# Retention attention and two MLPs on one core: POOL loads the decay matrix, chunks load in halves, w_in tiles move to the first pass

## What is computed

```python
for b in range(nb):                       # blocks of 64 tokens
    intra = (qb @ kb.T * Dmask) @ vb      # Dmask[i, j] = lam ** (i - j) for i >= j
    inter = (qb * lam_pow) @ kv_state
    out[:, :, sl] = intra + inter
    kv_state = lam_block * kv_state + (kb * rev_pow).T @ vb
x = out                                   # (1536, 512)
h = x @ w_in;  g = np.maximum(0.01 * h, h);  x = g @ w_out
out = ((x @ w1) * (x @ w2)) @ w3 @ moe2_w_out
```

## Time and profile before

| | |
|---|---|
| median of 3 runs | 555.33 us (554.99 to 555.40) |
| the profiled execution | 555.02 us, span 553.1 us |
| PE busy | 546.3 us (99%), 2930 matmuls |
| DVE, ACT, POOL busy | 192.1, 155.4, 31.4 us |
| granted clock of PE | 1.00 |
| attention | to about 91 us of the span |
| moved by DMA | 39.7 MB |

### The profile page before, as it was taken

How to read it: one execution, slowest core, us unless ns; L and a number is a source line. 1 busy time by engine, 2 the same in 40 slices (tenths; PEclk the granted TensorE clock), 3 DMA queues, 4 the chain that set the end, 5 groups by cost and what they waited for, 6 DMA issues and landing times.

```text
span 553.1 us, 7821 instructions
## 1 busy us (share of the span) xinstructions
PE 546.3 (99%) x2930; PEld 448.6 (81%) x2930; DVE 192.1 (35%) x295; ACT 155.4 (28%) x267; POOL 31.4 (6%) x42
## 2 busy tenths in 40 slices
PE   8999999999999999999999999999999999999997
PEld 6788887888888888888888888788888888888885
DVE  4585664544342422222534444311111111111111
ACT  5232423434232322222433433311112111130111
POOL 6332420000000000000000000000000000000000
PEclk9999999999999999999999999999999999999999
DMA  7997773323111000000113210000002000020002
GB/s 267 361 370 261 242 274 115 115 89 102 57 39 38 1 0 0 0 0 0 30 47 99 92 39 0 1 1 1 0 1 76 0 0 0 0 77 0 1 0 76
DMA packets 17257, 39.71 MB, mean 72 GB/s; under 512 B 1856, under 2 KB 2888, under 8 KB 15696
## 3 DMA queue, kind: packets, MB, share of 16 engines
q1 hardware_dynamic: 15728, 29.63, 16.1%
q10 hardware_dynamic: 1472, 9.72, 4.7%
q0 software_dynamic: 32, 0.01, 0.0%
HBM read 34.10 MB, written 5.25 MB: 71 GB/s over the span
## 4 chain that ended last, share of the span: by engine, by line
PE 94%; DMA 2%; POOL 1%; DVE 1%; ACT 1%; issue 0%; SPq 0%; ACTq 0%
PE hid L629 16%; PE hid L630 16%; PE hid L631 16%; PE acc L629 13%; PE acc L630 13%; PE acc L631 13%; PE acc L716 2%; PE hid L665 2%; DMA stage<-weights 1%; PE acc L710 1%; POOL pow_row L328 1%; PE hid L730 1%; DMA pow_dram<-pow_row 0%; POOL pow_two L330 0%; DMA pow_two<-lam 0%
## 5 line engine op out<-in xcount | busy, mean ns | idle before, releaser
L629 PE MATMUL hid<-xy_hi,wa_hi 128*128 (+1 forms) x384 | 149.5, 389 | 0.0
L631 PE MATMUL hid<-xy_hi,wa_lo 128*128 (+1 forms) x384 | 149.4, 389 | 0.0
L630 PE MATMUL hid<-xy_lo,wa_hi 128*128 (+1 forms) x384 | 149.4, 389 | 0.0
L410 ACT ACTIVATE g<-hid 128x512 f32<-128x512 f32 (+1 forms) x72 | 43.1, 598 | 261.3 <-PE hid L631 261.3
L629 PE MATMUL acc<-g_hi,wb 128*128 128x512 f32 x286 | 111.4, 390 | 0.3 <-DVE g_lo L503 0.3
L630 PE MATMUL acc<-g_lo,wb 128*128 128x512 f32 x286 | 111.3, 389 | 0.0
L631 PE MATMUL acc<-g_hi,wb 128*128 128x512 f32 x286 | 111.3, 389 | 0.0
L629 PEld LDWEIGHTS hid<-xy_hi,wa_hi 128*128 128x128 f32 x384 | 72.1, 188 | 15.1 <-issue 0.2
L630 PEld LDWEIGHTS hid<-xy_lo,wa_hi 128*128 128x128 f32 x384 | 72.1, 188 | 15.0
L631 PEld LDWEIGHTS hid<-xy_hi,wa_lo 128*128 128x128 f32 x384 | 72.1, 188 | 14.9
L568 DVE TENSOR_TENSOR g<-g,hid 128x512 f32<-128x512 f32 (+1 forms) x48 | 33.0, 687 | 122.2 <-ACT g L410 122.2
(11 more groups left out here) (75 smaller groups left out, 298.8 us busy)
## 6 DMA issues: line engine op xcount, KB each, us to landing
stage<-weights SPq DMA_DIRECT2D x72, 256.0 KB, 2.8
qkv<-attn ACTq DMA_DIRECT2D x9, 1024.0 KB, 6.2
qkv<-attn SPq DMA_DIRECT2D x3, 1024.0 KB, 7.3
outT<-stage SPq DMA_DIRECT2D x11, 256.0 KB, 2.1
stage<-w_dram SPq DMA_DIRECT2D x8, 256.0 KB, 2.6
w_dram<-g SPq DMA_DIRECT2D x4, 256.0 KB, 3.3
w_dram<-w_out SPq DMA_DIRECT2D x4, 256.0 KB, 3.5
decay<-pow_dram SPq DMA_DIRECT2D x1, 512.0 KB, 4.1
```

The lines of the kernel that those rows point to most:

```text
L410: nc.scalar.mul(g[:, n % 2, :], hid[:, n % 2, 0, :], factor).then_inc(scaled, 1)
L629: nc.tensor.matmul(out, w_hi, a_hi, start=first, stop=False)
L630: nc.tensor.matmul(out, w_hi, a_lo, start=False, stop=False)
L631: return nc.tensor.matmul(out, w_lo, a_hi, start=False, stop=final)
```

## The change

It has three parts. POOL waits for its own store of the powers and issues the load of `decay`; SP neither waits for it nor issues the load. A chunk comes in two loads, its transposed q and k (`q_and_k_loaded`) and its k and v (`values_loaded`), and those who read one part wait for that one; SP's written order takes the halves between the weights. And `W_IN_AT` puts 3 tiles of w_in into attention, behind chunks 9, 10 and 11, in place of 8, behind chunks 3 to 10; 13 are left to the first pass.

```diff
-W_IN_AT = [0, 0, 0, 1, 1, 1, 1, 1, 1, 1, 1, 0]
+W_IN_AT = [0, 0, 0, 0, 0, 0, 0, 0, 0, 1, 1, 1]
...
+        def chunk_parts(c):
+            u = c % ATTN_RING
+            return [(qkv[:, u, QT:KC, :], attn[c][:, QT:KC, :], q_and_k_loaded[u]),
+                    (qkv[:, u, KC:VC + 1, :], attn[c][:, KC:VC + 1, :], values_loaded[u])]
...
-            def load_chunk(c):
-                sp.dma_start(qkv[:, c, :, :], attn[c]).then_inc(chunk_loaded[c], 16)
-
-
-            for w in range(STAGE - 1):
+            def load_part(c, part):
+                to, source, loaded = chunk_parts(c)[part]
+                sp.dma_start(to, source).then_inc(loaded, 16)
+
+
+            before_scores = len(w34_tiles(0, FIRST_34))
+            for w in range(before_scores):
                 load_weight(w)
-            load_chunk(0)
-            for w in range(STAGE - 1, len(EARLY_34)):
+            load_part(0, 0)
+            for w in range(before_scores, len(EARLY_34)):
                 load_weight(w)
-            wait_then_step(pow_stored, 16)
-            every_shift = bass.AP(pow_dram, 0, [[1, P], [2 * CHUNK, H], [1, CHUNK]])
-            sp.dma_start(decay[:, :, :], every_shift).then_inc(decay_loaded, 16)
-            load_chunk(1)
+            load_part(0, 1)
+            load_part(1, 0)
             next_block = len(EARLY_34) + len(tiles_at(0))
             for w in range(len(EARLY_34), next_block):
                 load_weight(w)
-            load_chunk(2)
+            load_part(1, 1)
+            load_part(2, 0)
+            load_part(2, 1)
...
             pool.dma_start(pow_dram.ap(), pow_row[:, :]).then_inc(pow_stored, 16)
+            pool.wait_ge(pow_stored, 16)
+            every_shift = bass.AP(pow_dram, 0, [[1, P], [2 * CHUNK, H], [1, CHUNK]])
+            pool.dma_start(decay[:, :, :], every_shift).then_inc(decay_loaded, 16)
...
-                pool.wait_ge(chunk_loaded[u], 16 * (c // ATTN_RING + 1))
+                pool.wait_ge(values_loaded[u], 16 * (c // ATTN_RING + 1))
...
                 if c % CPB > 0:
+                    pool.wait_ge(q_and_k_loaded[u], 16 * (c // ATTN_RING + 1))
...
-                    act.dma_start(qkv[:, c % ATTN_RING, :, :], attn[c + ATTN_RING]).then_inc(chunk_loaded[c % ATTN_RING], 16)
+                    for to, source, loaded in chunk_parts(c + ATTN_RING):
+                        act.dma_start(to, source).then_inc(loaded, 16)
...
-                pe.wait_ge(chunk_loaded[u], 16 * (c // ATTN_RING + 1))
+                pe.wait_ge(q_and_k_loaded[u], 16 * (c // ATTN_RING + 1))
...
                 pe.wait_ge(masked, 2 * c + 2)
+                pe.wait_ge(values_loaded[u], 16 * (c // ATTN_RING + 1))
```

More of the change, by code:

```diff
@@ L180, in build @@
         q_pow_copied = sem("q_pow_copied")
-        chunk_loaded = [sem(f"chunk_loaded{i}") for i in range(ATTN_RING)]
+        q_and_k_loaded = [sem(f"q_and_k_loaded{i}") for i in range(ATTN_RING)]
+        values_loaded = [sem(f"values_loaded{i}") for i in range(ATTN_RING)]
         staged = [sem(f"staged{i}") for i in range(STAGE)]
```

## The result

The changed kernel takes 561.47 us (median of 4 runs, 561.31 to 562.05) against 555.27 us for the kernel before in the same comparison: a ratio of 1.0117, 95% interval 1.0101 to 1.0133. It is 1.2% slower. Its profiled execution took 561.33 us with a span of 559.2 us, 6.1 us more than before. "No change" was wrong, and the range ended at 560.0.

A forecast was written before the change was run, and what follows sets the result against it. PE's busy time bounds the kernel (546.3 of 553.1 us), with one 1.04 us stall in reach. The terms, -1.04 + 0.88 = -0.16 us, carried to the median of 555.33, gave 555.2 us, range 554.1 to 560.0.

The forecast's parts named there:

- No change: Whole kernel: the verdict that a measurement would not tell it from the kernel before, about 0.2% (1.1 us); chance 0.48.
- Part 1: SP no longer waits for the powers, so PE's whole stall before product 16 goes: -1.04 us.
- Part 2: POOL issues the decay load; it lands at 18.85 and stalls PE before chunk 0's value products: +0.88 us.
- The store: POOL's store of the powers to DRAM, ahead of the decay load: taken to land at 13.45 as before.
- The start: Fixed part of POOL's decay load besides its transfer: 2.7 us, as POOL's nearly empty store took.
- the share: Decay load beside SP's queue: an even share of bytes, 0.52 MB at half of 396 GB/s, 2.65 us.
- The clock: PE's granted clock: a stall of several us could lower it; not priced, left in the upper end.
- my formula: PE's stall before chunk 0's value products equals the decay landing less 17.97, one for one; with it -1.04 us.
- Rival 2: Decay load crawls piece by piece behind SP's rows, stalling PE: up to +6.1 us, 561.4 us; chance 0.27.
- Rival 3: POOL writes the decay load's 1024 pieces slowly: 4.3 us, +0.8, 556.1 us; at 8 us 559.8; chance 0.15.
- Part 3: Chunks loaded in halves, with more loads on SP and ACT and pieces of 4 instead of 8 KB: 0.
- Part 4: Five w_in tiles leave attention for the first pass, PE waiting for neither: 0.

The follow-up runs named there:

- a2: The kernel before with only the w_in tiles moved (3 in attention, 13 in the first pass): 554.93 against 554.95 us, ratio 0.9999.
- d1: The kernel before with weight 10 loaded ahead of chunk 1, behind the decay load on SP: 554.33 against 554.86 us, ratio 0.9994 (0.9985 to 1.0003).
- f1: The kernel before with POOL issuing the decay load and SP held until it has landed: 559.91 us in a single execution.
- b4: The changed kernel with ACT, behind its first ten hi parts, issuing the decay load in place of POOL: 564.9 us (1.0156 to 1.019).
- a4: The kernel before with only the chunks in halves, decay load still on SP: 559.03 us (1.0054 to 1.0095).
- c3: a4 with each half stored in one piece in DRAM: 554.77 against 554.86 us, ratio 1.0001 (0.999 to 1.0012).
- b1: The changed kernel with SP held for the powers' store before it loads q and k of chunk 1: 558.52 us.
- b2: The changed kernel with SP held for the powers' store only before k and v of chunk 1: 563.39 us.

## Why the prediction was wrong

**Part 1 was right in direction.** No wait for `w_ring` is left at 22 us, the engines are full from 12 to 15 us (408 GB/s), and weight 10 lands by 16.6 (I had counted about 13, but no product wanted it before 22). But its 1.04 us was the size in one trace. How early PE is differs from trace to trace: its matmuls on the powers start anywhere between 10.95 and 11.85 us in 14 traces of different kernels. Before, product 16 waited for a tile that came by its own clock, so a later start only shortened that wait: a2 starts 0.67 us later than before and waits 0.2 instead of 1.04. d1's half microsecond fits that: what PE waits in one trace is not all to be had.

**Part 2 is the step that failed.** I put the landing at 18.85; it was 23.04. The 4.19 us divide like this.

- *The store.* I took it as landing at 13.45 as before. It was issued 1.08 us sooner and still landed later, so the decay load went out at 15.15 instead of 13.51: 1.64 us. The store is itself a transfer of POOL's queue and waits beside SP's transfers. The earlier trace rows had hinted at it: the engines ran dry at 12 us and the store landed at 13.4. f1, whose store was issued 1.7 us earlier than before's, landed it no earlier. I had priced a load behind a full queue and forgotten the store ahead of it.
- *The start.* My fixed part was 2.7 us, taken from a store that itself had met little backlog at its end. From issue to landing the load took 7.9 us, 2.65 of them the transfer that I had priced; the other 5.2 are mostly the wait of 4.2 us until its first data, which is 1.6 us through idle engines (f1). 2.5 us of the miss.
- *The pace was right, the share was not even.* Some 0.5 MB moved in about 2.7 us from the first data, with pieces of 4 KB. From 20 to 22 us POOL's queue had 0.40 MB and SP's 0.23: more than half, of engines that together moved less (313 GB/s, not 396). The two errors cancel in my 2.65 us, which is luck. The Trainium skill ("DMA: Bandwidth & Descriptors", Queues, rings and completion order) says that an engine alternates between queues by packets; the counts of 107 and 121 agree. Its section SWDGE vs HWDGE vs iDMA gives packets of preferably up to 4096 B for GpSimd's queue; 3.7 KB on average agrees. Alternation alone would have let the load start as soon as in f1; in the trace it starts 2.6 us later, and no run shows what it waits for there.

**The clock was named and left out of the sum.** The prediction said that a long stall could lower it and that no row showed one, and so priced it at nothing. It costs 2.1 us of the 6.1. With the landing of 23.04 alone my formula gives 5.07 - 1.04 = 4.0 us, 559.3 us, inside the range; the clock took it out.

**Rival 2 gave 561.4 us and the time was 561.47, which is luck.** Its landing was 25.1, with 1024 small pieces served one by one for 8.9 us; the trace has 23.04, with 128 pieces of 4 KB served in 2.7 us behind a late store and a late start. Its stall is 2 us too long, and the clock, which it left out, costs 2. b4 shows the mechanism that I had described, on another queue. Rival 3 is out: the issue took 0.97 us, and in f1 the data flowed 1.6 us after it.

**Part 3 was right in this kernel only by cover.** a4 shows that halves cost 4 us where the decay load is in time, because of rows 8 KB apart (c3). I had noted that pieces shrink to 4 KB and looked no further. **Part 4** was right: a2.

## What to carry to other kernels

A load that is short and urgent should stay on the queue that carries the bulk, ahead of it. On another queue it does not overtake the bulk at once: its first data came 3.3 to 4.5 us after the issue wherever SP was loading too, even where SP had only just begun, and the store that it depends on was late in the same way. So count that wait for every link of the chain. A wait of a few us on PE costs its own length and then, where the granted clock falls, half a clock until it returns: about two more in this kernel.

## What the runs showed of the hardware

- A load on a second queue beside SP's transfers got its first data 4.2 us after its issue in the changed kernel, 3.3 in b1, 4.5 in b2 and 3.7 on ACT's queue in b4; in f1, with idle engines, 1.6. The trace of before had shown it too: ACT's first chunk load was issued at 21.51, got its first data at 25.0 and took 8.7 us to land.
- The same 512 KB, read in runs of 512 B, goes out as pieces of 4 KB on POOL's queue and of 512 B on SP's and ACT's.
- 4 KB rows that lie 8 KB apart ran at 214 to 255 GB/s in the first loads and near 400 later; the same rows stored together ran at 382 to 404 at once.
- PE's granted clock fell to 0.50 about 2.3 us into a stall (20.1 to 22.4) and returned at 29.2, some 4.8 us after PE had work again.
